# The guard's sum, product and flag inside the last pass, its load ahead of the end, and the last store in three parts

## What is computed

```python
def _attn_ref(r, k, v, w, u):            # 4 batches, 8 heads, 768 tokens, 48 channels
    for t in range(S):
        cur = np.einsum('bhd,bhe->bhde', u[None] * kt, vt)
        y[:, :, t] = np.einsum('bhd,bhde->bhe', rt, state + cur)
        state = wt[:, :, :, None] * state + np.einsum('bhd,bhe->bhde', kt, vt)
def _moe_ref(x, w_in, w_out, g_ln):      # 384 -> 1024 -> 384
    h = x @ w_in
    solu = h * softmax(h)
    ln = (solu - mean(solu)) / np.sqrt(var(solu) + 1e-06) * g_ln
    return ln @ w_out
def _moe2_ref(x, w_in, w_out):           # 384 -> 2048 -> 384
    h = x @ w_in
    return np.maximum(0.01 * h, h) @ w_out
```

## Time and profile before

| | |
|---|---|
| median of 3 runs | 805.15 us (804.94 to 806.25) |
| the profiled execution | 804.72 us, its span 802.7 us |
| busy in the span | PE 782.0, PEld 736.1, DVE 533.8, ACT 344.5, POOL 178.3 us |
| mean granted TensorE clock | 0.996 |
| the last stage | from 744.95 us, PE's last matmuls from 794.37 us |
| the last store issued | 796.78 us |

### The profile page before, as it was taken

One profiled execution on the slowest core, in us unless ns is written; L12 is line 12 of the kernel. 1 busy time (PEld: TensorE's weight loads), 2 busy tenths in 40 slices (PEclk: granted clock), 3 DMA queues, 4 the chain that ended last, 5 costly groups with the idle time before them and its releaser, 6 DMA issues.

```text
span 802.7 us, 12113 instructions
## 1 busy us (share of the span) xinstructions
PE 782.0 (97%) x4624; PEld 736.1 (92%) x4624; DVE 533.8 (66%) x1023; ACT 344.5 (43%) x676; POOL 178.3 (22%) x199
## 2 busy tenths in 40 slices
PE   5999999999999999999999999999999999999996
PEld 4769988899999999999999999999999999999996
DVE  6788989865668657667666676576675765553332
ACT  3386554444344343353443444345334444334332
POOL 4524313222213302222212122122221221100000
PEclk9999999999999999999999999999999999999999
DMA  9940222032021121030220311203202020000000
GB/s 274 324 173 5 62 65 65 1 94 65 1 65 39 56 65 35 30 94 1 65 65 1 95 31 34 65 1 94 65 1 65 16 79 30 1 0 30 1 1 33
DMA packets 19377, 45.88 MB, mean 57 GB/s; under 512 B 1920, under 2 KB 14336, under 8 KB 18928
## 3 DMA queue, kind: packets, MB, share of 16 engines
q1 hardware_dynamic: 15664, 37.17, 15.5%
q10 hardware_dynamic: 3648, 7.87, 2.9%
HBM read 40.31 MB, written 4.72 MB: 56 GB/s over the span
## 4 chain that ended last, share of the span: by engine, by line
PE 79%; DVE 1%; ACT 0%; issue 0%; DVEq 0%; ACTq 0%
PE BANKS L1138 55%; PE MISC L1138 20%; PE BANKS L1317 2%; PE MISC L1162 1%; PE MISC L1155 1%; DVE att L827 0%; DVE Rraw L967 0%; DVE RL L974 0%; ACT RH L697 0%; ACT Rraw L693 0%; DVE ki L835 0%; DVE X2L L991 0%; DVE A L848 0%; ACT X2H L714 0%; ACT OUT L720 0%
## 5 line engine op out<-in xcount | busy, mean ns | idle before, releaser
L693 ACT ACTIVATE Rraw<-BANKS 128x384 f32<-128x384 f32 x128 | 63.0, 492 | 217.7 <-PE BANKS L1138 217.5
L967 DVE TENSOR_TENSOR Rraw<-BANKS,Rraw 128x384 f32<-128x384 f32 x128 | 71.1, 555 | 118.8 <-ACT Rraw L693 118.7
L1138 PE MATMUL BANKS<-RH,W4H 128*128 128x384 f32 x384 | 136.1, 354 | 0.9 <-DVE RL L974 0.8
L1138 PE MATMUL BANKS<-X2H,W3H 128*128 128x384 f32 x384 | 130.7, 340 | 0.2 <-DVE X2L L991 0.2
L1138 PE MATMUL BANKS<-RH,W4L 128*128 128x384 f32 x384 | 129.8, 338 | 0.0
L1138 PE MATMUL BANKS<-RL,W4H 128*128 128x384 f32 x384 | 129.5, 337 | 0.0
L1138 PE MATMUL BANKS<-X2L,W3H 128*128 128x384 f32 x384 | 129.4, 337 | 0.0
L1138 PE MATMUL BANKS<-X2H,W3L 128*128 128x384 f32 x384 | 129.2, 336 | 0.0
L697 ACT ACTIVATE RH<-Rraw 128x384 fp32r<-128x384 f32 x128 | 67.2, 525 | 94.3 <-DVE Rraw L967 94.3
L974 DVE TENSOR_TENSOR RL<-Rraw,RH 128x384 fp32r<-128x384 f32 x128 | 79.3, 619 | 22.5 <-ACT RH L697 22.5
L835 DVE RECIPROCAL ki<-att 112x128 f32<-112x128 f32 x96 | 89.4, 938 | 0.0
(11 more groups left out here) (132 smaller groups left out, 1490.0 us busy)
## 6 DMA issues: line engine op xcount, KB each, us to landing
att<-rkw SPq DMA_DIRECT2D x23, 672.0 KB, 5.0
out<-OUT SPq DMA_DIRECT2D x8, 576.0 KB, 6.4
rtok<-r_tok SPq DMA_DIRECT2D x22, 192.0 KB, 4.8
ktok<-k_tok SPq DMA_DIRECT2D x22, 192.0 KB, 4.6
vtok<-v_tok SPq DMA_DIRECT2D x22, 192.0 KB, 4.9
W3raw<-w_in ACTq DMA_DIRECT2D x1, 3072.0 KB, 18.0
W4raw<-w_out ACTq DMA_DIRECT2D x1, 3072.0 KB, 17.3
W1raw<-w_in SPq DMA_DIRECT2D x2, 768.0 KB, 11.2
```

The costliest lines, as they stand in the source:

```text
L693: nc.scalar.activation(Rraw[:, fp % 2, :], PR[fp % 2][:, 0:ST], ACT.Copy, scale=0.01).then_inc(act_slope, 1)
L967: nc.vector.tensor_tensor(Rraw[:, fp % 2, :], PR[fp % 2][:, 0:ST], Rraw[:, fp % 2, :], ALU.max).then_inc(dve_relu, 1)
L1138: return nc.tensor.matmul(dst, lhsT, rhs, start=start, stop=stop, skip_group_check=True)
```

## The change

- DVE's sum and comparison move from the end into the last M2 stage, ahead of step 2; the flag's write moves ahead of step 8. PE's 1x1 product moves ahead of step 5.
- PE, DVE and ACT load the flag ahead of step 13 and keep it in a register; at the end they only branch. POOL's load is where it was in its own program, behind the wait for the flag.
- The last super block is stored in three DMAs of 192 KB, each issued when its activation is done, the first two with a semaphore of their own, `stored_parts`.
- SP waits for the stores behind its load and branch, not ahead of them.

```diff
+        def closing(b, kind, so):
+            return isinstance(b, int) and b == B - 1 and so == SPB - 1 and kind == "M2"
...
-                if last:
+                if last and isinstance(b, int) and b == B - 1:
+                    for m in range(KM):
+                        sp.wait_ge(act_out, supers(b, SPB - 1, KM, m + 1))
+                        sp.dma_start(out[bass.ds(supers(b, SPB - 1) * 128, 128), m * ST:(m + 1) * ST],
+                                     OUT[:, m, :]).then_inc(stored if m == KM - 1 else stored_parts, 16)
+                elif last:
                     store(b, SPB - 1, first_row)
...
             body(B - 1, True)
-            sp.wait_ge(stored, 16 * NST)
...
                 sp.wait_ge(stored, 2 * 16 * NST)
+            sp.wait_ge(stored_parts, 16 * (KM - 1))
+            sp.wait_ge(stored, 16 * NST)
...
         def _(act):
+            def read_flag():
+                act.wait_ge(guarded, 1)
+                wild.append(act.value_load(flag[0:1, 0:1], min_val=0, max_val=1))
...
+                    if closing(b, kind, so) and f == F2 - 3:
+                        read_flag()
...
-            act.wait_ge(guarded, 1)
-            with act.If(act.value_load(flag[0:1, 0:1], min_val=0, max_val=1) > 0):
+            with act.If(wild[0] > 0):
...
         def _(dve):
+                    if closing(b, kind, so) and f == 2:
+                        judge()
+                    if closing(b, kind, so) and f == 8:
+                        raise_flag()
+                    if closing(b, kind, so) and f == F2 - 3:
+                        read_flag()
...
         def _(pe):
+                    if closing(b, kind, so) and f == F2 - 3:
+                        read_flag()
+                    if closing(b, kind, so) and f == 5:
+                        pe.wait_ge(judged, 4)
+                        mm(TB[0:1, 0:1], tame[:, :], ones[:, :], True, True).then_inc(pe_tame, 1)
...
-            pe.wait_ge(judged, 4)
-            mm(TB[0:1, 0:1], tame[:, :], ones[:, :], True, True).then_inc(pe_tame, 1)
...
-            pe.wait_ge(guarded, 1)
-            with pe.If(pe.value_load(flag[0:1, 0:1], min_val=0, max_val=1) > 0):
+            with pe.If(wild[0] > 0):
```

More of the change, by code:

```diff
@@ L247, in build @@
         ld_w = [sem(f"ld_w{i}") for i in range(4)]
-        stored = sem("stored")
+        stored, stored_parts = sem("stored"), sem("stored_parts")
         consts, chain = sem("consts"), sem("chain")
@@ L720, in take_out @@
                     nc.scalar.activation(OUT[:, m, :], ACC[m][:, 0:ST], ACT.Copy).then_inc(act_out, 1)
+            wild = []
+            def read_flag():
+                act.wait_ge(guarded, 1)
+                wild.append(act.value_load(flag[0:1, 0:1], min_val=0, max_val=1))
             def run(b, listed, item=item, attend=True):
                 for kind, so, f, fp, items in listed:
+                    if closing(b, kind, so) and f == F2 - 3:
+                        read_flag()
                     out_due = kind == "M1" and not (isinstance(b, int) and b in (0, B) and so == 0)
@@ L992, in take_x2, with judge, raise_flag, read_flag @@
                                             ALU.subtract).then_inc(dve_x2, 1)
+            def judge():
+                dve.wait_ge(act_range, 2 * NCH)
+                nc.vector.tensor_reduce(total[:, :], spread[:, :], AX.X, ALU.add).then_inc(judged, 1)
+                dve.wait_ge(judged, 3)
+                nc.vector.tensor_scalar(tame[:, :], total[:, :], LIMIT, None, ALU.is_le).then_inc(judged, 1)
+            def raise_flag():
+                dve.wait_ge(pe_tame, 1)
+                nc.vector.tensor_scalar(flag[0:1, 0:1], TB[0:1, 0:1], PD - 0.5, None, ALU.is_lt).then_inc(guarded, 1)
+            wild = []
+            def read_flag():
+                dve.wait_ge(guarded, 1)
+                wild.append(dve.value_load(flag[0:1, 0:1], min_val=0, max_val=1))
             def run(b, listed, item=item, attend=True):
                 for kind, so, f, fp, items in listed:
+                    if closing(b, kind, so) and f == 2:
[4 more added lines that the diff above has]
+                        read_flag()
                     m, s = items[0]
@@ L1089, in _ @@
             run(B - 1, batch_steps(True))
[L1092 to L1097, removed]
             def channel(i, e):
@@ L1113, in channel @@
                 nc.vector.tensor_tensor(GM[:, :], GR[:, :], GKV[:, :], ALU.mult).then_inc(gdve, 1)
-            dve.wait_ge(guarded, 1)
-            with dve.If(dve.value_load(flag[0:1, 0:1], min_val=0, max_val=1) > 0):
+            with dve.If(wild[0] > 0):
+                dve.wait_ge(stored_parts, 16 * (KM - 1))
                 dve.wait_ge(stored, 16 * NST)
@@ L1348, in cons, with read_flag @@
                 last.then_inc(pe_cons, 1)
+            wild = []
+            def read_flag():
+                pe.wait_ge(guarded, 1)
+                wild.append(pe.value_load(flag[0:1, 0:1], min_val=0, max_val=1))
             def run(b, listed, item=item):
```

## The result

The changed kernel takes 802.78 us (median of 9 runs, 801.61 to 806.04) against 805.15 (9 runs), a ratio of 0.9968 with a 95% interval of 0.9956 to 0.9979: 2.4 us less, against 802.8 forecast. The profiled execution took 802.3 us with a span of 800.2, against 804.72 and 802.7. The sum was nearly met, but not by its own terms, as the rows show.

A forecast was written before the change was run, and what follows sets the result against it. PE's late, slow branch was taken to bound the end. ACT's arrival at 799.9 plus 0.3 barrier plus 0.2 product gave 800.4 instead of 802.7, 2.3 us less: 802.8 us on the median, range 801.8 to 804.5.

The forecast's parts named there:

- What bounded the kernel: At the closing barrier PE came last, at 802.4 us, its 4851 ns branch waiting for code behind the store's packets.
- The product: PE's 1x1 product ahead of step 5, uncovered: +0.2 us, bounds 0.1 and 0.35.
- The flag's loads: Early loads ahead of step 13: 0.75 to 0.9 us each, covered by idle time or queued matmuls, costing nothing.
- The emptied queue: Rival: PE's early load lets its matmul queue run dry, costing 1.3 us, 804.15 us; chance 0.11.
- the lost clock: Rival: a gap from PE's load also drops the clock, +1.7 us, 805.85 us; chance 0.04.
- PE's branch: At the end, PE branches between 794.9 and 795.9 us instead of 797.5 and is no longer last at the barrier.
- the late branch: Rival: PE branches only at its last matmul, 796.1 us, at full old cost; gain 1.2, 803.95 us; chance 0.07.
- ACT's branch: At the end, ACT branches at 796.3 us instead of 797.3; DRAIN at 799.9, floor 799.1, ceiling 800.6, last arrival.
- the wait of a part or more behind the first part's packets: ACT's code queues behind store parts: DRAIN at 799.5, or one part later 800.0, instead of the floor's 799.1.
- the fetch behind the whole store: Rival: ACT's code comes only behind the third part, about 798.4 us; gain 1.5, 803.65 us; chance 0.12.
- The store in three: Last store's parts issued about 795.8, 796.3, 796.8 us; third lands after 2.8 us (bounds 2.4, 3.3), at 799.6.
- SP: SP's load and branch run while parts fly; only DRAIN, 0.1 us instead of 1.3, follows landing; arrival 799.7.

The follow-up runs named there:

- Experiment 1: Kernel before, with only SP's wait for its stores moved behind its flag load and branch: 804.74 us, ratio 0.9999.
- experiment 2: Changed kernel with one whole last store and SP waiting for it ahead of its load, as before: 804.2 us, ratio 0.9983.
- experiment 7: Changed kernel with PE loading the flag five times at step 13 instead of once: 803.31 us, one execution.
- Experiment 6: Kernel before with the last super block's store left out: 803.1 us, one execution, against 804.39 for the kernel before beside it.
- experiment 4: Kernel before with only the last super block's store split in three: 804.0 us, ratio 0.9972.
- experiment 5: Kernel before, writing the last 576 KB once more to scratch ahead of the last store: 810.49 us, one execution.
- experiment 3: Changed kernel with the last super block stored whole, SP still waiting behind its branch: 802.87 us, ratio 0.9972.
- experiment 9: Changed kernel with sum and comparison in the stage before, product ahead of the last M2's first step, and the last store whole: 802.64 us, ratio 0.9965.
- the repeated runs: Changed kernel run again, unedited, beside the kernel before: 802.98 us, ratio 0.9971, 2.0 us under the kernel before.
- experiment 8: Changed kernel with sum and comparison in the stage before and the product ahead of the last M2's first step, where PE waits anyway: 802.23 us, ratio 0.9967.
- experiment 10: Changed kernel with the product in a gap PE has anyway, and ACT issuing the third store part ahead of its branch: 803.23 us, ratio 0.9978.

## Why the prediction was right, step by step

**What bounded the kernel** held: PE's branch, with ACT and DVE beside it. Experiment 1 shows it, as SP's earlier arrival alone brings nothing, and experiment 2, as SP comes last once the branches are early. The early loads of PE, DVE and ACT were never taken one by one, so what each is worth alone is not shown.

**The product** was mis-sized: 0.2 us taken, 0.32 measured, near the bound of 0.35. The step that failed was to scale the three transposes of the earlier trace rows by their small size; two one-column passes cost as much.

**The flag's loads** on ACT, DVE and PE, DVE's sum, comparison and flag: nothing, as forecast. PE's spacing at step 13 is unchanged, and experiment 7 puts the sequencer's lead at 2.9 us, close to the 3 us of the earlier trace rows. The emptied queue (0.11), and the lost clock that rested on it (0.04), fall.

**PE's branch** started at 794.33 and its DRAIN was at 797.9: "before 796, and no longer the last" holds, and the late branch (0.07) falls. PE arrives 4.5 us sooner: 3.1 us of that is the earlier start of the branch, 1.35 its shorter length. So the traffic was less than a third of the old price, and the 3.5 us that are left are paid even by a branch alone. Experiment 6 adds that about 1 of the 1.35 us was the company of the other engines' code and not the store, which the prediction had not seen.

**ACT's branch** came at 796.16 (forecast 796.3) but its DRAIN at 798.96 instead of 799.9. That is the floor of 2.8 us to a tenth, though composed otherwise: 0.9 us from branch to packet instead of 0.5, and 1.9 from packet to DRAIN instead of 2.3. The step that failed is the wait of a part or more behind the first part's packets; there was none to be seen. So the fetch behind the whole store (0.12) falls for this kernel, while the kernel before against experiment 4 (2.0 us from ACT's branch to the code, and 0.95 once the store ended sooner) and experiment 5 show that its mechanism is there, when the fetch meets a store in full flight.

**The store in three** landed at 799.78, 3.0 us behind the third issue, instead of 799.6 and 2.8. The third part took 3.0, 2.7, 2.7 and 2.6 us in the four kernels that have parts and SP's early branch, so the 2.8 chosen between the bounds of the earlier trace rows was sound. The step that failed is the other side: the whole store's 3.4 us were held fixed, and it landed after 3.1 in experiments 3 and 9 (3.4 again in experiment 2). And the parts pay for their issues: the second took 0.5 to 0.7 us instead of 0.34, more than a copy lasts, so that the third was issued 0.95 to 1.1 us behind the start of the last large matmul, the whole store 0.89.

**SP** therefore is last, not ACT. From landing to DRAIN it is 0.24 us, not 0.1 (a second branch of 38 ns stands in between), and the release 0.2 instead of 0.3.

Sum, with the measured terms: last arrival 800.0 instead of 799.9, barrier 0.2 instead of 0.3; the product of 0.32 is in the 800.0 already. The end came at 800.2 against 800.4. That the number was hit is in part luck, twice over. First, the sum named the wrong engine. Counted from the start of the last large matmul it had ACT arrive after 4.0 us and SP after 3.8; measured were 3.2 and 4.2. ACT was 0.8 us too late in the sum and SP 0.4 too early, and the later of the two came out nearly right. Second, the span and the first median carry the upstream 0.4 us; without it the change is worth 2.0 us, as the repeated runs say, against 2.3 forecast. (The chances of the forecast add up to 1.01, with the 0.01 for causes not seen.)

## What to carry to other kernels

A branch whose taken side is not loaded cost microseconds at the end of this kernel (3.5 to 5.2 on PE), and least where its engine took it early and alone: load its condition some steps ahead, and let the engine go straight from its last instruction into the branch. Where several engines arrive at a barrier within a microsecond of each other, change them together: SP's edit alone showed nothing and the guard's alone 1 us, where both gave 2.3. And do not put one more issue ahead of a branch that has little slack. A short operation without cover on a full engine belongs into a gap that the engine has anyway.

## What the runs showed of the hardware

- From a branch to the first packet of its code it was 0.92 to 1.04 us on PE and ACT in the changed kernel and in experiments 2, 3, 4, 6, 8 and 9. With a store in the way it was 1.9 to 2.0 us in the kernel before and in experiment 1, 1.5 for ACT in experiment 10, and 2.1 (ACT) and 3.7 (PE) with the store doubled. PE's 16 KB packet took 1.0 to 1.2 us alone and 1.6 to 2.0 us beside those of other engines. The whole branch of PE took 3.50 to 3.75 us ahead of the store, 4.45 with all engines at once, 4.85 and 5.23 with the whole store besides, and 6.15 with the store doubled. The Trainium skill (Advanced Engine Details and Errata, Control Flow Timing) gives a compare-and-branch about 108 ns; the instruction by itself is recorded with 50 ns on ACT, whose wait for code comes behind it. By the packets the rest was the fetch and the time until the engine went on.
- The large matmuls of the last stage stood 0.1734 us apart in some executions and 0.1766 in others, at a granted clock of 1.00 in both; over the stage that is 0.9 us, three times what the product cost. It did not go with the kernel: the changed one had a mean of 0.1742 in its first trace, and 0.1766 when run again. The cause is open.
- The clock fell at 155 us in only 3 of the 13 profiled executions: for 3.4 us in the kernel before and in experiment 10, for 6.8 us in experiment 5. The window 150 to 160 us (us, busy of PE, PEld, DVE, ACT, POOL, clock, DMA share, GB/s), in the kernel before and in that of experiment 1:

```profile
150.00:160.00 10.00, 8.55 (x52) 8.18 (x51) 9.62 (x15) 2.99 (x7) 3.66 (x4) 0.83 0.01 2
```

```profile
150.00:160.00 10.00, 8.29 (x59) 7.51 (x59) 10.00 (x16) 4.29 (x9) 3.73 (x4) 1.00 0.01 2
```

The two kernels are the same there. A mean of 0.83 is the lower level (1.2 GHz) for a third of the window, and PE gets through 52 matmuls instead of 59. This and the spacing are why a tail in a trace tells more of such a change than the whole time of one execution.
